# Attention and a Sinkhorn-weighted expert layer on one core: one Sinkhorn normalization a step, the second products in four runs

## What is computed

```python
logits = x @ w_gate
logits = logits - logits.max()
P = np.exp(logits)
for _ in range(8):
    P /= P.sum(1, keepdims=True) + 1e-09
    P /= P.sum(0, keepdims=True) + 1e-09
    P *= N / E
for e in range(E):
    h = np.maximum(x @ w1[e], 0.0)
    ye = h @ w2[e]
    out += P[:, e:e + 1] * ye
```

## Time and profile before

| | us |
|---|---|
| median of 3 runs | 1628.05 |
| lowest, highest | 1627.33, 1628.24 |
| the profiled execution | 1627.57 |
| its span, first to last instruction | 1625.8 |
| PE busy in the span | 1595.2 |
| PEld (weight loads of PE) busy | 1426.5 |
| POOL busy | 998.5 |
| DVE busy | 732.0 |
| ACT busy | 543.2 |

### The profile page before, as it was taken

How to read it: one execution, slowest core, us unless ns; L and a number is a source line. 1 busy time by engine, 2 the same in 40 slices (tenths; PEclk the granted TensorE clock), 3 DMA queues, 4 the chain that set the end, 5 groups by cost and what they waited for, 6 DMA issues and landing times.

```text
span 1625.8 us, 24296 instructions
## 1 busy us (share of the span) xinstructions
PE 1595.2 (98%) x8880; PEld 1426.5 (88%) x8880; DVE 732.0 (45%) x1264; ACT 543.2 (33%) x774; POOL 998.5 (61%) x645
## 2 busy tenths in 40 slices
PE   7888999999999999999999999999999999999999
PEld 6877888888898888889888898888889888898888
DVE  5757634434434434434434344344344344344343
ACT  4742232332323333233232332334323333233331
POOL 5975555656556777565656656677565655656552
PEclk9999999999999999999999999999999999999999
DMA  7611212122121213212112121122211212122111
GB/s 216 180 54 52 74 56 78 52 77 75 54 77 52 77 52 117 78 52 78 65 64 77 52 77 63 66 77 91 78 62 68 78 52 77 57 72 77 52 65 39
DMA packets 34157, 120.41 MB, mean 74 GB/s; under 512 B 3904, under 2 KB 4160, under 8 KB 34112
## 3 DMA queue, kind: packets, MB, share of 16 engines
q1 hardware_dynamic: 34112, 119.80, 21.5%
HBM read 115.06 MB, written 4.72 MB: 74 GB/s over the span
## 4 chain that ended last, share of the span: by engine, by line
PE 94%; POOL 3%; DVE 2%; issue 1%; ACT 0%; POOLq 0%; DVEq 0%
PE ps L456 17%; PE ps L455 16%; PE ps L457 16%; PE ps L439 14%; PE ps L435 14%; PE ps L437 14%; POOL probs L756 1%; POOL sc L748 1%; PE ps L356 0%; PE ps L345 0%; PE ps L333 0%; DVE prob L1010 0%; DVE row_sum L985 0%; PE ps L502 0%; POOL t_raw L737 0%
## 5 line engine op out<-in xcount | busy, mean ns | idle before, releaser
L714 POOL TENSOR_TENSOR w_lo<-w_raw,w_hi 128x1792 fp32r<-128x1792 f32 (+2 forms) x98 | 391.0, 3990 | 529.5 <-ACT w_hi L548 529.4
L597 ACT ACTIVATE h_hi<-ps 128x384 fp32r<-128x384 f32 x384 | 189.0, 492 | 961.8 <-DVE ps L887 450.3
L456 PE MATMUL ps<-w_lo,h_hi 128*128 128x512 f32 x1152 | 457.0, 397 | 0.0
L457 PE MATMUL ps<-w_hi,h_lo 128*128 128x512 f32 x1152 | 456.6, 396 | 0.0
L455 PE MATMUL ps<-w_hi,h_hi 128*128 128x512 f32 x1152 | 455.3, 395 | 1.3 <-POOL w_lo L721 1.3
L439 PE MATMUL ps<-xv_hi,w_lo 128*128 128x384 f32 x1344 | 452.6, 337 | 0.0
L435 PE MATMUL ps<-xv_hi,w_hi 128*128 128x384 f32 x1344 | 450.8, 335 | 1.4 <-DVE logits L965 1.4
L437 PE MATMUL ps<-xv_lo,w_hi 128*128 128x384 f32 x1344 | 450.0, 335 | 0.0
L869 DVE SCALAR_TENSOR_TENSOR h_lo<-ps,h_hi 128x384 fp32r<-128x384 f32 x384 | 214.1, 558 | 361.6 <-ACT h_hi L597 360.9
L435 PEld LDWEIGHTS ps<-xv_hi,w_hi 128*128 128x128 f32 x1344 | 253.3, 188 | 31.4 <-DVE logits L965 1.5
L437 PEld LDWEIGHTS ps<-xv_lo,w_hi 128*128 128x128 f32 x1344 | 253.2, 188 | 29.1
(11 more groups left out here) (75 smaller groups left out, 948.1 us busy)
## 6 DMA issues: line engine op xcount, KB each, us to landing
w_raw<-w SPq DMA_DIRECT2D x192, 512.0 KB, 3.9
qk_buf<-qk SPq DMA_DIRECT2D x16, 576.0 KB, 5.5
v_win<-v SPq DMA_DIRECT2D x16, 288.0 KB, 4.3
out<-x_raw SPq DMA_DIRECT2D x18, 256.0 KB, 2.6
const_sb<-consts SPq DMA_DIRECT2D x1, 176.0 KB, 3.5
wg<-w_gate SPq DMA_DIRECT2D x1, 64.0 KB, 4.3
```

The source lines that it names most:

```text
L456: nc.tensor.matmul(ps_y[t], h_hi[slot][:, f, c], w2_lo[slot][:, f, :], start=False, stop=False)
L457: last = nc.tensor.matmul(ps_y[t], h_lo[slot][:, f, c], w2_hi[slot][:, f, :], start=False, stop=closes)
L597: nc.scalar.activation(h_hi[slot][:, f, half * HT:(half + 1) * HT], o, ACT.Relu)\
L714: last = nc.gpsimd.tensor_tensor(w1_lo[:, slot, c], w1_raw[:, slot, (lo + 1) * BLK:(hi + 1) * BLK], w1_hi[:, slot, c].bitcast(F32), ALU.su ...
```

## The change

The text of the diff, in words:

- `RUNS` gives the 12 halves of a step to four places: none after P1, two after P6 (t = 0), none after P2, two after P7 (t = 1), none after P5, six after P4 (t = 2, 3, 4), two after P3 (t = 5). It holds for all 95 windows.
- One Sinkhorn iteration a step: `spread_columns(n - 1)` stands after P4 of step `n`, for `n` = 1 to 8. On DVE the end of iteration `n - 1` and the rows of iteration `n` stand in one piece after `rest(..., 2)` and ahead of `add_c12`. PE waits before P1 of the next step for the rows' end (`col_part_ready`), and in step 1 before P4.
- `row_sum`, `row_inv`, `col_sum`, `col_inv` lie in PSUM, in the free 128 columns of the bank `1 - slot`.
- `max_diag` is made by ACT. DVE no longer subtracts the maximum but negates it (one value a partition), and ACT's Exp adds it as its bias.
- The wait for `logits_out` stands before the first half of t = 5 in step 1, not before P1.
- ACT's first `w2_split` moves from behind step 0's last relu to ahead of the last `v_shift`.
- Expert 0 of block 0 is copied unweighed to `acc` in step 4; in step 8, when `P` is final, ACT weighs its six tiles (`weigh_first`, ahead of `relu_12`), and DVE's first five takes of expert 1 come after iteration 7 and each after the weighing of its tile (`first_weighed`).
- The written-out part reaches to step 11.

```diff
+RUNS = [(0, 0), (0, 2), (2, 2), (2, 4), (4, 4), (4, 10), (10, 12)]
...
-        row_sum = sb(ctx, "row_sum", [P, NT])
-        row_inv = sb(ctx, "row_inv", [P, NT])
...
+        col_sum = [a[:, 0:E] for a in spread]
+        col_inv = [a[:, E:2 * E] for a in spread]
+        row_sum = [a[:, 2 * E:2 * E + NT] for a in spread]
+        row_inv = [a[:, 2 * E + NT:2 * E + 2 * NT] for a in spread]
...
+                if isinstance(n, int) and n == 0 and t == TT - 1 and f == 0:
+                    pe.wait_ge(logits_out, 1)
...
-                for k, (lo, hi) in enumerate([(0, 2), (2, 4), (4, 6), (6, 8), (8, 10), (10, 11), (11, 12)]):
+                for k, (lo, hi) in enumerate(RUNS):
+                    if columns and k == P1:
+
+                        pe.wait_ge(col_part_ready, columns + 1)
                     if top and k == P7:
                         pe.wait_ge(max_all_ready, 1)
-                    if after_p6 is not None and k == P7:
-                        pe.wait_ge(chain, after_p6 * 8 + 5)
-                    if after_p7 is not None and k == P5:
-                        pe.wait_ge(chain, after_p7 * 8 + 5)
+                    if top and k == P4:
+                        pe.wait_ge(col_part_ready, 1)
...
-                    if after_p4 is not None and k == P4:
-                        spread_columns(after_p4, 1 - slot)
+                    if columns is not None and k == P4:
+                        spread_columns(columns, 1 - slot)
...
-            pe.wait_ge(logits_out, 1)
...
+            def max_spread_out():
+                act.wait_ge(max_part_out, 1)
+                nc.scalar.activation(max_diag[:], ident, ACT.Copy, scale=max_part[:, 0:1]).then_inc(max_part_ready, 1)
+
+            def weigh_first():
+
+                act.wait_ge(chain, SINKHORN * 8)
+                for t in range(TT):
+                    act.wait_ge(y_taken, t + 1)
+                    o = acc[:, 0, t * DM:(t + 1) * DM]
+                    at = place(0, t)
+                    nc.scalar.activation(o, o, ACT.Copy, scale=prob[:, at, 0:1]).then_inc(first_weighed, 1)
...
                 relu_21(n, slot)
+                if isinstance(n, int) and n == SINKHORN:
+                    weigh_first()
                 relu_12(n, slot)
...
             exp(NP - 1)
+            w2_split(16, 0, 0)
             v_shift(NP - 1)
...
             relu_12(0, 0)
-            w2_split(16, 0, 0)
+            max_spread_out()
...
                 add_c22(n, slot)
+                if sinkhorn is not None:
+                    dve.wait_ge(col_sum_ready, sinkhorn + 1)
+                add_c21(n, slot)
                 rest(n, slot, bank[slot], 1, 1, 1)
...
                 rest(n, slot, bank[1 - slot], 1, 0, 2)
+                if sinkhorn is not None:
+                    columns(sinkhorn, 1 - slot)
+                    if not final:
+                        row_sums(sinkhorn + 1, 1 - slot)
+                        rows(sinkhorn + 1, 1 - slot)
+                some(0 if final else 2, 5)
                 add_c12(n, slot)
...
                 rest(n, slot, bank[slot], 0, 1, 3)
-                if after_p4 is not None:
-                    rows(after_p4 + 1)
-                some(4, 6)
+                some(5, 6)
```

More of the change, by code:

```diff
@@ L194, in build @@
         y_taken = sem("y_taken")
+        first_weighed = sem("first_weighed")
         out_done = sem("out_done")
@@ L681, in _ @@
                         window(n, landed(n), j)
-                with act.Fori(1, E - 1) as e:
+                if s == 0:
+                    for n in range(FP, 3 * FP):
+                        window(n, landed(n), n % FP)
+                with act.Fori(1 if s else 3, E - 1) as e:
                     for j in range(FP):
@@ L899, in take @@
                 dve.wait_ge(y_done, done + (t + 1))
+                if s == 0 and isinstance(e, int) and e == 1:
+                    dve.wait_ge(first_weighed, t + 1)
                 o = acc[:, s, t * DM:(t + 1) * DM]
@@ L903, in take @@
                 weight = flat[:, at:at + 1] if isinstance(at, int) else flat[:, bass.ds(at, 1)]
-                if first:
+                if first and s == 0:
+                    nc.vector.tensor_copy(o, ps_y[t]).then_inc(y_taken, 1)
+                elif first:
                     nc.vector.tensor_scalar(o, ps_y[t], weight, None, ALU.mult).then_inc(y_taken, 1)
@@ L907, in take, with window @@
                     nc.vector.scalar_tensor_tensor(o, ps_y[t], weight, o, ALU.mult, ALU.add).then_inc(y_taken, 1)
-            def window(n, j, takes=None, top=False, after_p6=None, after_p7=None, after_p4=None):
+            def window(n, j, takes=None, top=False, sinkhorn=None):
                 slot = j % 2
-                last = after_p6 == SINKHORN - 1
+                final = sinkhorn == SINKHORN - 1
                 def some(lo, hi):
@@ L919, in some @@
                             take(*takes[:3], t, takes[3])
-                if after_p6 is not None:
-                    dve.wait_ge(col_sum_ready, after_p6 + 1)
                 if top:
```

120 lines of the change are left out of this document (46 added, 74 removed).

## The result

The changed kernel takes 1607.55 us (median of 4 runs, 1606.69 to 1609.14) against 1628.14 us for the kernel before (1627.33 to 1629.39) on the same chip: a ratio of 0.9874, 95% interval 0.9857 to 0.9891. Forecast were 1606.3 us in a range of 1602.5 to 1613.5. The profiled execution took 1607.48 us, with a span of 1605.7 us: 20.1 us less than the profiled execution before, where the sum had 21.3.

A forecast was written before the change was run, and what follows sets the result against it. PE's matmuls were taken to bound the kernel (busy 98% of the span), with waits and a lower clock in the Sinkhorn steps. Sum: 1627.57 - 16.1 (Sinkhorn part) - 6.1 (runs) + 0.9 (steps 32, 64) = 1606.3 us; range 1602.5 to 1613.5.

The forecast's parts named there:

- Start: Before step 1: without the wait for the logits, its P1 starts 1.40 us earlier, at 106.81 us.
- Step 1: In step 1: the spread of the maximum and P6's wait for a late quarter of step 0 add 0.6 us.
- Placing: Sinkhorn iteration behind P4 on DVE: nothing late in steps 1 to 3 and 5 to 7, cover 1.1 us.
- Step 4: Three takes of 0.74 us behind DVE's iteration in step 4 make P6 of step 5 late by 0.5 us.
- Step 8: ACT's first weighing and five DVE takes in step 8 make the last quarter late by 1.05 us.
- The four runs: Steps 9 to 95: fewer slow first halves shorten the steady step 0.07 us to 15.59, 6.1 us in all.
- steps 32 and 64: P5 of these two steps comes due before DVE's rest is done: 0.45 us each, 0.9 us added.
- PSUM operands, no change: DVE's Sinkhorn operands in PSUM: iteration time taken as unchanged; within 0.1 us per instruction the total moves under 1 us.
- rival that POOL would hold DVE up all the same: Sinkhorn steps: PSUM operands don't free DVE from POOL, some 0.3 us a step, 1608.5 us; chance 5%.
- the runs give nothing: Steady steps: a step with four runs still takes 15.66 us, total 1613 us; chance 17%.
- slower rival: P6 binds in all 95 steps if the last quarter comes over 0.55 us later; at 1 us, 1649 us; chance 4%.
- rival of a dip at the start: Around step 1: PE's clock falls once all the same, step 1 loses 3.5 us, total 1609.8 us; chance 12%.

The follow-up runs named there:

- the floats behind one of the two tiles: Changed kernel with 52 unused floats a partition allocated behind w2_hi0 and w2_lo0, so h and the odd w2 pair move: 1609.8 us, ratio 0.9884.

## Why the prediction was right, step by step

It held in total and nearly everywhere in its parts. By its own steps, forecast to measured (changed kernel):

| step of the prediction | forecast | measured | on the sum |
|---|---|---|---|
| *Start*: P1 of step 1 | 106.81 | 107.72 | +0.91 |
| *Step 1*, over 15.84 | 0.6 | 0.63 | 0.0 |
| *Placing*: cover | 1.1 | 1.18 | 0.0 |
| *Step 4*: P6 of step 5 late | 0.5 | 0.15 | -0.35 |
| *Step 8*: P6 of step 9 late | 1.05 | 1.18 | +0.13 |
| *The four runs*: steady step | 15.59 | 15.60 | +0.9 |
| steps 32 and 64, each | 0.45 | 0.28 | -0.34 |

The last column adds to +1.2, the distance from -21.3 to -20.1.

- *Start.* The wait of 1.40 us went, and step 0 took 17.02 us (forecast 17.11). But step 0 itself began 1.00 us later. That is the attention part, which the change hardly touches: over the profiled runs of all kernels here step 0 begins at 89.3 to 91.8 us, and with w2's split back at its old place at 90.67. The term was right, its origin varies.
- *Step 9 begins at 235.7*: 235.16. Here the text made a slip: the stop of 1.05 us before P6 lies inside step 9, not ahead of it. In the total it counts once either way.
- *Step 4 and step 8.* The takes of the changed kernel ahead of the last quarter, in step 4, then in step 8:

```profile
169.23 1.87 DVE L925 COPY x_raw<-ps 128x512 f32<-128x512 f32 x3
```

```profile
232.01 3.62 DVE L929 SCALAR_TENSOR_TENSOR x_raw<-ps,prob,x_raw 128x512 f32<-128x512 f32 x5 [0.91 <-ACT x_raw L636]
```

  In step 4 expert 0 is copied and not weighed, and the forecast priced the copies with the weighed take of the earlier trace rows: 3 x 0.74 = 2.22 us in place of 1.87. This is the term that was sized wrongly. P6 of step 5 was then only 0.03 us late, and the slow restart of 0.11 us, which the term left out, made it 0.15. In step 8 the weighed takes need 0.72 us each and P6 of step 9 was late by 1.07 us, forecast 1.05; with the restart that makes the 1.18.
- *Steps 32 and 64.* The forecast's own terms add to 6.14 + 0.07 - 5.90 + 0.1 = 0.41 us, not 0.45. Measured were 0.17 of stop and 0.11 of restart. The relu there starts 0.09 us before ACT's w1 split ends (601.13 against 601.22) and not 0.08 behind it as in the earlier trace rows.
- *PSUM operands, no change.* An iteration takes 2.51 us against 2.47, and L1008 0.16 from PSUM. The figure of 120 against 58 fixed cycles from the Trainium skill (VectorE: DVE Perf Modes, the TRN2 errata) would have made it 0.45 longer, by an estimate from that page; the rows don't show that. The rival that POOL would hold DVE up all the same didn't occur.
- *The four runs.* The mechanism of the forecast, the slow first half behind a product, is what this kernel shows: pairs 1.391, six halves 4.137 us. Undone, the step is 15.66 again. The Trainium skill (TensorE: Matmul & The Clock Gate, "Wait — 56ns, not 53.3ns?") gives 216 ns from start to start for 512 columns; no kernel here shows that, 227 ns was the shortest mean over a run of halves. (A slip of the recorded sum: seven products of 1.04 us leave 8.38 of 15.66 us, not 8.36. It lies within the bounds given there.) But the forecast took the distances of the old trace for a property of the order. They are one of the order and of the tiles' places in SBUF together, and the change moved the tiles. At the old places the same order gives 15.54. The step that failed in kind is thus that *the four runs* were priced with no thought for the SBUF tiles that went, and it did little harm by luck: with all tiles moved together, the steps tried lie between 15.54 and 15.65, which over steps 9 to 95 gives -10.4 to -0.6 us in place of -5.2. At 15.65 the rival *the runs give nothing* would have had its time, for another reason than its own.
- *P6.* The margin holds in every steady step, and one half less takes 28.6 us. The forecast's 0.55 us less one half of 0.70 gives a stop of 0.15; measured were 0.20 and 0.11 for the slow restart. So the margin was read within 0.05 us. The recorded price of the slower rival left the restart out, though: by its rule of 95 stops alone, a stop of 0.20 us would have cost 19 us and not 28.6.
- *Clock.* 1.00 from step 1 to the end of the steady part. Even the kernel with w2's late split, where PE was idle 1.25 us in step 1, stayed at 1.00 there. In the old order it fell in step 1 even with POOL cut short in steps 2 and 3: 0.92 in the first of the two windows shown there. The rival of a dip at the start is nearer than the changed kernel's own trace shows: in some kernels with its order the clock fell to the 1.2 GHz level at the end of the attention part and stayed there into step 0. With the floats behind one of the two tiles step 0 was granted 0.94 and took 17.97 us, with w2's late split 0.96 and 17.72 us, where the changed kernel has 1.00 and 17.02.

**What each part was worth.** From step 0's start to step 9's the profiled runs took 162.05 us before (251.75 - 89.70) and 144.46 after: 17.6 us less: 5.6 in steps 0 and 1, 12.7 in steps 2 and 3, and 0.75 given back in steps 4 to 8, which now have an iteration each. Shortening POOL's instructions alone gives the kernel before 11.5 of those 12.7: they are the lock and the waits and clock dips behind it. w2's split is worth 3.1. The new order with the sums still in SBUF takes 147.2 us from step 0 to step 9, so the order and the split give 14.8 of the 17.6. The sums in PSUM save 3.35 us in steps 1 to 9, and cost 5.5 us through the places of the tiles: by itself, this part of the change lost. The wait for the logits and the maximum on ACT were not undone alone; what each is worth isn't shown.
